# Loads of weights moved from ACT's program to SP's, behind a block's two transfers; y rows a quarter at a time; one PE wait moved

## The reference, cut to what matters

```python
for t in range(S):                                   # gated linear attention, 4 x 8 heads, 768 steps, 48 wide
    state = alpha[:, :, t, :, None] * state + einsum(k[:, :, t], v[:, :, t])
    y[:, :, t] = einsum(q[:, :, t], state)
x = y as (3072 tokens, 384)
expert_idx = argmax(normalized(x) @ normalized(expert_emb).T / tau, axis=1)     # one of 8 experts
for e in range(8):                                   # "the first network"
    out[mask] = gate_w[mask, None] * (maximum(x[mask] @ w1[e], 0) @ w2[e])      # 384 -> 1024 -> 384
h = out @ w_in                                       # "the second network", 384 -> 2048 -> 384
return maximum(0.01 * h, h) @ w_out
```

## Time and profile before

| | |
|---|---|
| median of 3 runs | 835.44 us (835.06 to 837.01) |
| the profiled execution's own time | 839.64 us |
| its span, first to last instruction | 837.9 us |
| PE busy | 808.3 us (96%) |
| granted TensorE clock, mean | 0.991 |

### The profile page before, as it was taken

The page is one execution under the profiler, slowest core; times in us unless marked ns, Lnnn a source line. Parts: engine busy times, 40 slices in busy tenths (PEclk is TensorE's granted clock), DMA queues, the critical chain, the costliest instruction groups (busy, mean ns, idle before and its releaser), DMA issues.

```text
span 837.9 us, 16982 instructions
## 1 busy us (share of the span) xinstructions
PE 808.3 (96%) x5267; PEld 725.0 (87%) x5268; DVE 451.2 (54%) x703; ACT 347.3 (41%) x643; POOL 203.1 (24%) x278
## 2 busy tenths in 40 slices
PE   7999999998999999996999999999999999999998
PEld 7888887987888998885989998998998998998997
DVE  7889986766656656653365433533532533443332
ACT  3545564635445446452344323323323333333223
POOL 6666623232333332332114003003003001000100
PEclk9999999999999999999899999999999999999999
DMA  9998664686788689789313201201101001000001
GB/s 230 251 261 241 201 217 135 213 280 218 267 277 281 226 269 276 266 268 245 132 5 40 38 1 39 38 1 38 23 16 38 0 0 38 1 1 5 33 1 38
DMA packets 63449, 107.84 MB, mean 129 GB/s; under 512 B 24167, under 2 KB 45203, under 8 KB 63408
## 3 DMA queue, kind: packets, MB, share of 16 engines
q1 hardware_dynamic: 47312, 67.25, 28.2%
q10 hardware_dynamic: 10208, 25.23, 8.9%
q0 software_dynamic: 5888, 14.85, 5.6%
HBM read 78.37 MB, written 30.32 MB: 130 GB/s over the span
## 4 chain that ended last, share of the span: by engine, by line
PE 79%; DMA 6%; DVE 5%; issue 4%; ACTq 2%; ACT 1%; DVEq 1%; POOL 1%; SPq 1%; POOLq 0%
PE bank L1608 24%; PE bank L1653 24%; PE bank L1581 11%; PE bank L1561 8%; DMA hidden_rows<-hs 3%; PE bank L1403 3%; PE bank L1443 2%; PE bank L1420 2%; DMA hds<-hidden_rows 2%; PE bank L1451 1%; PE bank L1409 1%; DVE wts L422 1%; DVE hT L1306 1%; PE bank L1463 1%; ACTq L430 1%
## 5 line engine op out<-in xcount | busy, mean ns | idle before, releaser
L1608 PE MATMUL bank<-yT,wts 128*128 128x512 f32 x864 | 217.2, 395 | 0.9 <-DVE ys L1357 0.9
L1653 PE MATMUL bank<-wts,gs 128*128 128x384 f32 x1152 | 215.4, 335 | 0.4 <-ACT os L940 0.2
L1653 PEld LDWEIGHTS bank<-wts,gs 128*128 128x128 f32 x1152 | 202.1, 188 | 10.7 <-issue 1.6
L1608 PEld LDWEIGHTS bank<-yT,wts 128*128 128x128 f32 x864 | 160.7, 188 | 31.8 <-issue 1.2
L1220 DVE TENSOR_TENSOR g<-bank,small 128x512 f32<-128x512 f32 x96 | 66.4, 692 | 175.3 <-ACT small L854 167.3
L1581 PE MATMUL bank<-wts,hT 128*128 x744 | 141.4, 346 | 16.4 <-DVE hT L1306 16.1
L1581 PEld LDWEIGHTS bank<-wts,hT 128*128 128x128 f32 x744 | 132.6, 194 | 18.8 <-issue 18.5
L854 ACT ACTIVATE small<-bank 128x512 f32<-128x512 f32 x96 | 57.6, 600 | 186.0 <-PE bank L1608 167.4
L1561 PE MATMUL bank<-wts,gxT 128*128 (+1 forms) x549 | 131.5, 392 | 0.1
L1561 PEld LDWEIGHTS bank<-wts,gxT 128*128 128x128 f32 x549 | 102.3, 188 | 20.7 <-issue 0.5
L1370 DVE TENSOR_TENSOR gs<-g,gs 128x512 fp32r<-128x512 f32 x96 | 66.6, 693 | 66.3 <-ACT gs L951 60.7
(11 more groups left out here) (175 smaller groups left out, 705.9 us busy)
## 6 DMA issues: line engine op xcount, KB each, us to landing
raw<-weights ACTq DMA_DIRECT2D x48, 512.0 KB
hidden_rows<-hs SPq DMA_DIRECT2D x28, 512.0 KB
hds<-hidden_rows SPq DMA_DIRECT2D x28, 512.0 KB
qkas<-qka SPq DMA_DIRECT2D x20, 675.5 KB, 7.0
raw<-weights SPq DMA_DIRECT2D x12, 512.0 KB
vs<-v SPq DMA_DIRECT2D x24, 192.0 KB, 5.9
x_rows<-xs SPq DMA_DIRECT2D x24, 192.0 KB, 4.1
yl<-y_rows SPq DMA_DIRECT2D x20, 192.0 KB
```

The source lines that it names most:

```text
L1608: m = pe.matmul(gps[f % 2][:, :], wts[:, 0, w_part, n:n + P], yT[:, 1 - u, y_part, k], start=(k == 0 and (w_part, y_part) == (0, 0)), stop ...
L1653: m = pe.matmul(ops[tt], gs[:, f % 4, g_part, tt * P:(tt + 1) * P], wts[:, 1, w_part, f * D:(f + 1) * D], start=(f == 0 and (g_part, w_par ...
```

## The change

- SP issues the loads of weights. `load_next(m)` comes behind the two transfers of block m (`move`): it reads `wtab`, and where block m - 1 is the first of its expert it loads half 0, where block m - 3 is, half 1. These are the loads that ACT issued in step m - 2. One load, W1 of expert 2, comes ahead of block 2's store. ACT keeps only the code for the last steps, in which no load falls due with these inputs.
- SP's code for blocks 2 to 5 and 20 to 29 is written out; blocks 6 to 19 are a loop.
- y rows of groups 0 and 1 are loaded a quarter at a time, behind blocks 20 to 23 and 26 to 29.
- PE's wait for `ys_ready` (and for the last split of W1's half) stands in the first `outward` instead of ahead of the loop.

```diff
+            def load_next(m):
+                if isinstance(m, int) and m == FIRST:
+                    with sp.If(sp.snap(table(sp, 0) & (2 * E)) > 0):
+                        load_half(sp, 0, 3)
+                    return
+                code = table(sp, m - 3)
+                last_first, third_first = sp.snap(code & (4 * E)), sp.snap(code & E)
+                with sp.If(last_first > 0):
+                    load_half(sp, 0, sp.snap((table(sp, m - 1) & (E - 1)) + 2))
...
+                    with sp.If(third_first > 0):
+                        load_half(sp, 1, sp.snap((code & (E - 1)) + 2))
+            def move(w, u):
+                move_h(w, u)
+                load_next(w)
...
-            for u in range(2):
-                move_h(FIRST + u, u)
-            move_pairs(FIRST // 2 + 1, 10)
-            load_y(0, 0)
-            move_pairs(10, 13)
-            load_y(1, 1)
-            move_pairs(13, WINDOWS // 2)
+            sp.wait_ge(tables_ready, 2)
+            load_half(sp, 0, 2)
+            for w in range(FIRST, FIRST + 4):
+                move(w, w % 2)
+            with sp.Fori(FIRST // 2 + 2, 10) as i:
+                for u in range(2):
+                    move(i * 2 + u, u)
+            for w in range(20, MOVED):
+                move(w, w % 2)
+                if w in (20, MOVED - QUADS):
+                    wait_rows(w // (MOVED - QUADS))
+                if w < 20 + QUADS:
+                    load_quarter(0, w - 20)
+                elif w >= MOVED - QUADS:
+                    load_quarter(1, w - MOVED + QUADS)
...
-                if ahead(w, 1):
-                    with act.If(first1 > 0):
-                        load_half(act, 0, act.snap((table(act, w + 1) & (E - 1)) + 2))
...
-                elif not (isinstance(w, int) and w == 0):
+                if isinstance(w, int) and w >= MOVED - 2:
...
                     with act.If(first_front > 0):
                         load_half(act, 1, act.snap((table(act, w - 1) & (E - 1)) + 2))
...
             def outward(t, u, f):
                 s = t * FT + f
                 pe.wait_ge(g_lo, s + 1)
+                if u == 0 and f == 0:
+                    pe.wait_ge(ys_ready, WINDOWS)
+                    pe.wait_ge(w_lo[0], SET_OUT * 3 + 3)
...
-            pe.wait_ge(ys_ready, WINDOWS)
-            pe.wait_ge(w_lo[0], SET_OUT * 3 + 3)
```

More of the change, by code:

```diff
@@ L360, in head_rows @@
             return slice(64 * r, 64 * r + HD)
-        FIRST = 2
+        FIRST, MOVED = 2, WINDOWS - 1
         def turns_by_pe(w):
@@ L370, in by_squares @@
         def by_squares(w):
-            return not (isinstance(w, int) and (w < FIRST or w == WINDOWS - 1))
+            return not (isinstance(w, int) and (w < FIRST or w >= MOVED))
         def passed(w, u):
@@ L537, in move_h, with wait_rows @@
                 sp.dma_start(hds[:, u].rearrange("p (i n) -> p i n", i=QUADS), h_quarters[u]).then_inc(h_moved[u], 16)
-            def move_pairs(start, end):
-                with sp.Fori(start, end) as i:
-                    for u in range(2):
-                        move_h(i * 2 + u, u)
-            def load_y(t, u):
+            def load_next(m):
[7 more added lines that the diff above has]
+                    load_half(sp, 0, sp.snap((table(sp, m - 1) & (E - 1)) + 2))
+                if isinstance(m, int) and m == FIRST + 1:
+                    with sp.If(sp.snap(code & (2 * E)) > 0):
+                        load_half(sp, 1, 2)
+                elif isinstance(m, int) and m == FIRST + 2:
+                    load_half(sp, 1, sp.snap((code & (E - 1)) + 2))
+                else:
+                    with sp.If(third_first > 0):
+                        load_half(sp, 1, sp.snap((code & (E - 1)) + 2))
+            def move(w, u):
+                move_h(w, u)
+                load_next(w)
+            def wait_rows(t):
                 newest = min(t * TG + 2 * TG - 1 + E - 1, WINDOWS - 1)
@@ L550, in load_y, with load_quarter @@
                     sp.wait_ge(yt_turned, (t - 1) * KD)
[L552 to L561, removed]
-                move_h(FIRST + u, u)
-            move_pairs(FIRST // 2 + 1, 10)
-            load_y(0, 0)
-            move_pairs(10, 13)
-            load_y(1, 1)
-            move_pairs(13, WINDOWS // 2)
+            def load_quarter(t, j):
+                u = t % 2
+                if t == GROUPS - 1:
+                    for tt, tile in enumerate(LATE_TILES):
+                        sp.dma_start(yl[j * SQ:(j + 1) * SQ, u, tt * P // SQ:(tt + 1) * P // SQ],
+                                     y_late[tile, j]).then_inc(yl_in[u], 16)
+                    return
+                sp.dma_start(yl[j * SQ:(j + 1) * SQ, u],
+                             y_blk[t:t + 1, j].rearrange("a r n d -> (a r) n d")).then_inc(yl_in[u], 16)
+            sp.wait_ge(tables_ready, 2)
[13 more added lines that the diff above has]
+                    load_quarter(1, w - MOVED + QUADS)
             for j in range(2):
@@ L571, in _ @@
             for t in range(2, GROUPS):
-                load_y(t, t % 2)
+                wait_rows(t)
+                for j in range(QUADS):
+                    load_quarter(t, j)
             for tt, tile in enumerate(LATE_TILES):
@@ L865, in step @@
                         first_weights(0, 1)
-                        load_half(act, 0, 2)
                         first_weights(1, 2)
@@ L882, in step @@
                     gx_round(w + 3, 1 - u)
-                if isinstance(w, int) and w == 0:
-                    with act.If(act.snap(2 * E - first1) > 0):
-                        load_half(act, 0, 2)
-                if ahead(w, 1):
-                    with act.If(first1 > 0):
-                        load_half(act, 0, act.snap((table(act, w + 1) & (E - 1)) + 2))
[L890 to L894, removed]
-                elif not (isinstance(w, int) and w == 0):
+                if isinstance(w, int) and w >= MOVED - 2:
+                    if ahead(w, 1):
+                        with act.If(first1 > 0):
+                            load_half(act, 0, act.snap((table(act, w + 1) & (E - 1)) + 2))
                     with act.If(first_front > 0):
```

## The result

The change made the kernel slower: 843.39 us (840.96 to 844.99, 5 runs) against 836.63 (835.06 to 838.97, 5 runs) of the kernel before on the same chip, a ratio of 1.0077 (95%: 1.0049 to 1.0106). I had forecast 815.0, with 813 to 829 as the range. Where I quote a trace, it is one profiled execution; that of the changed kernel took 843.39 us itself.

What follows compares the result with a forecast made beforehand. PE, 96% busy, was held by late `hT`, the last `ys` and low clock. Gains 5.0 + 5.8 + 1.5 + 5.3 + 3.1 + 0.9 = 21.6 us, less 1.3 of new waits, took 835.44 to 815.1, rounded to 815.0; range 813 to 829.

Steps and rivals of the forecast that it cites:

- the queue's sum: SP's one queue, blocks 4 to 27: 5.5 us a block, 5.1 a load, 1.2 a y quarter; 1.3 us of new waits.
- part 2: Loads behind the block transfers: blocks 2, 4 and 25 give back 5.8 us, block 4's low clock 1.5 us.
- the slack of 7.8: How late a block's transfers may run before PE waits: 14.1 us from the store's issue less 6.3 us, 7.8 us.
- A: Rival: queue backlog longer than taken, 3 to 16 us of new waits at blocks 12 and 22 to 28; 818.5 to 831; chance 0.27.
- C: Rival: slower, each store behind 1.57 MB in one queue; over 21.6 us of new waits if a load exceeds 6.6; chance 0.10.
- L: Time of one load of weights in the queue, taken as 5.1 us, with 6.4 us as the upper end.
- the signs that I had named for being wrong: In the changed profile: PE waits growing from block 21 to 28 or at 6, 9, 12; splits awaiting loads; loads over 6 us.
- B: Rival: bytes cost the same anywhere, so waits of blocks 2, 4 and 25 stay with their clock; 821.1 us; chance 0.07.
- SP's new instructions: SP's table reads and three issues, some 0.5 + 3 x 0.5 us, cost nothing unless the backlog is there.
- Parts 3 and 4: y rows in quarters give 5.3 us of block 26's waiting and 3.1 of low clock; PE's moved wait gives 0.9.
- Part 1: Taking the load issues off ACT ends PE's waits at blocks 6, 9, 20 and 23: 5.0 us.
- ACT's splits: ACT's splits due some 16 us behind a block's store, loads landing 11.4 us behind it: no wait, 4 us of cover.

Runs made afterwards that it cites:

- e4: The changed kernel, with SP reading the table and working out its conditions while it waits for the store to land; 834.57 us.
- e9: e5 measured once more: the changed kernel with early table reads and each whole load directly behind its block's store; 815.53 us.
- e6: e1 with ACT issuing the same loads one step later, behind its rounding of the following block's h; 818.21 us.
- e10: e6 with the change's table reads and conditions put on SP behind each block's transfers, no DMA in them; 815.97 us.
- e1: The changed kernel with the loads left on ACT as before; y rows in quarters and PE's moved wait kept; 825.77 us.
- e7: The changed kernel with two more reads of the table ahead of each block's conditions on SP; 845.22 us.
- e5: The changed kernel with early table reads and the whole load directly behind the store, ahead of the wait for its landing; 816.57 us.

## Why the prediction was wrong

**The step that failed** is one term of the queue's sum in part 2, the load: "I take 5.1 us, since it was measured in this stage and with the transfers of blocks around it". In the changed kernel, turns without a load and without y rows took 5.54 us in the mean of six (5.2 to 6.0), and turns with a load and without y rows 12.28 us in the mean of twelve (11.1 to 13.4). So a load added 6.7 us to a turn, not 5.1. The other terms held: 5.54 us is the 5.5 that I had for a block, its 0.8 us hidden as I said, and the four turns with a quarter of y rows and no load took 6.78 us, 1.2 us more.

By packets, the 15 turns with a load (12.45 us in the mean, three of them with y rows) have 3.56 us from the load back's issue to its last packet, 6.10 more to the load's, 2.30 to the store's, and 0.49 to the next load back's issue. In the twelve without y rows the load's part is 6.03 us, and the store's 2.18, where a turn without a load has 1.52 from the load back's last packet to the store's: 0.7 us more, which no run explains. The 5.1 us of the earlier trace rows were packets that followed others without a gap: in the microsecond ahead of that window, 330.5 to 331.5 us in the trace before, the DMA ran at full rate:

```profile
DMA packets 183, 0.43 MB, mean 433 GB/s; under 512 B 15, under 2 KB 98, under 8 KB 183
```

In the new order the load starts slowly behind a load back. Its 21st packet of 384 starts 0.96 us after the load back's last, and from there to its end it is again 5.1 us. In e4, where the load is issued 0.9 us earlier, that 0.96 is 0.13. The earlier trace rows was also the kindest choice: in the trace of the kernel before, the eight loads that had q10 to themselves took 5.2 to 8.3 us from first to last packet.

With the measured term my own sum comes near the result: 9 x 5.5 + 6 x 6.7 = 89.7 against 78.3, 8 x 5.5 + 4 x 6.7 + 1.2 = 72.0 against 69.6, and 7 x 5.5 + 5 x 6.7 + 6.0 = 78.0 against 60.9 are 30.9 us behind, 23.1 over the slack of 7.8. I had 1.3; the trace has 25.0 with the low clock. Taken where the backlog is longest, it closes. From the load back of block 4 to that of block 12 (174.89 to 260.24) SP took 85.4 us for eight blocks, 15.8 more than 8 x 8.7; less the slack that is 8.0 us, and PE had lost 8.9 by then (7.4 of waits, 1.5 of low clock). From there to block 28 (415.16) it was 154.9 us for sixteen blocks, 15.7 more than 16 x 8.7, with no slack left, and PE lost 15.7 (11.4 of waits, 4.3 of low clock). The low clock was in no line of my sum, but by this account it didn't come on top: what PE lost, by waits or by clock, is what the queue fell behind.

**A and C.** A named part of the right blocks (12 and 22 to 28), with too small an L. C had the size: 841.4 us at L = 7 and "each store stands behind 1.57 MB in one queue". Its condition, L over 6.6 us, held by what a load added to a turn (6.7), though the load's own packets took 6.1. I read the slope (0.1 us of L counts 15 times) and then chose L from the most favourable row. A load of over 6 us in q1 and waits at blocks 6, 9 and 12 were among the signs that I had named for being wrong.

**B and the rule behind it.** The Trainium skill, "DMA: Bandwidth & Descriptors", section "Issuing engines are not separate DMA queues", says that DMAs of several engines end up on the same DMA engines, and that another issuing engine saves only the time to issue. Where nothing waits behind a load, the trace agrees: e9 has the loads in SP's queue and e6 in ACT's, with 815.53 and 818.21 us, and the queue matters little. But B, which I drew from it, is refuted: the waits of blocks 2, 4 and 25 are gone in the changed kernel, and the same bytes in the same queue at another place (e9) are worth 28 us. e6 and the change differ by 25 us, far more than three issues take (1.4 us), but since e6 also starts nine of its loads earlier, no run shows how much of this is the queue's.

**SP's new instructions** "cost nothing unless the backlog is there": the condition held, and the backlog was there. e10 shows the first half, e4 the second: 8.8 us of the loss (6.9 by ratios) are the load's late start. The remaining 19 (834.6 against e9's 815.5; 18 by ratios) are the order of store, load back and load.

**Parts 3 and 4** were right in size: e1 gives 9.6 us for 9.3 forecast. Part 1 has no run of its own. In e6 ACT still issues every load, a step later, and PE waits for `hT` only 2.2 us in all, so that the place of ACT's issues may have counted as much as their length. All parts together, with the backlog taken out by e9, give 815.5 where the sum without new waits was 835.44 - 21.6 = 813.8.

**ACT's splits.** I put their wait for loads at nothing, with 4 us of cover. In the changed kernel the page has 15.1 us of idle time ahead of the splits, 14.8 of it for loads. The timeline of ACT around the longest of these waits (4.78 us), in the step that ends with `hT` of block 9:

```profile
229.52 2.96 ACT L416 ACTIVATE wts<-raw 128x1024 f32 x3 [4.78 <-DMA raw<-weights]
234.38 1.15 ACT L860 ACTIVATE hT<-hds 128x512 fp32r<-128x512 f32 x2 [1.91 <-DMA hds<-hidden_rows]
```

The split is late, but `hds` came later still, so the backlog, not the load itself, held PE there. Without backlog the cover is real (0.0 in e9).

**Open:** why 1 us more in front of each load left the turn as it was (e7), when 1 us less shortened it by 0.8 (e4): the load's packets then begin to flow 1.5 us behind its issue instead of 2.4, and no run shows the reason.

## What to carry to other kernels

When a queue carries a chain of dependent transfers, price a new transfer in it by the whole turn, from one dependent issue to the next, with the empty stretches that the dependency leaves, and compare that with the period; if the margin is small against the spread of the durations that you have measured, take the sum at both ends before choosing, since an error counts once for each transfer. Then put the bulk transfer into the stretch in which the chain waits anyway: directly behind the store it costs nothing here, behind the load back it costs 28 us. Instructions in front of a bulk DMA can make it miss the end of the transfer ahead: taking them away gave 7 to 9 us here (e4).

## What the hardware showed that I had not expected

- A load back that starts into an empty queue takes 3.6 us from its issue to its last packet in the changed kernel, of which 1.1 pass before its first. In e9, where that of block 10 follows a load without a gap, nothing of this shows: packets flow at full rate from 231.0 to 232.9 us, and most of its 512 are among them. The transfer itself isn't shorter there: its last packet ends at 234.06, 3.2 us behind its first, when the next block's store is under way.

```profile
DMA packets 555, 0.70 MB, mean 371 GB/s; under 512 B 30, under 2 KB 502, under 8 KB 555
```

- One profiled execution (e5's) ran its matmuls at about twice their length for the whole kernel, 1591.6 us:

```profile
200.00:400.00 200.00, 199.99 (x558) 152.26 (x555) 76.02 (x146) 59.55 (x102) 34.87 (x47) 1.00 0.35 122
```

In e9's trace, of the same kernel, the same stretch has 1040 matmuls. The granted clock of 1.00 in this line is not a reading: the page of this execution has no PEclk row, and that of e9 has one. So a clock in the windows says something only where the page has that row. At which clock this execution ran, and why, isn't recorded.
